# Second mixture of a fused attention and two-mixture kernel: three alternations a pair instead of eight

## The reference, cut to what matters

```python
def _moe2_ref(x, domain_probs, w1, w2):            # x 1536 x 384, w1 4 x 384 x 1024, w2 4 x 1024 x 384
    p = domain_probs / (domain_probs.sum(-1, keepdims=True) + 1e-09)
    out = np.zeros((N, D), dtype=np.float32)
    for e in range(E):
        h = np.maximum(x @ w1[e], 0.0)
        out += p[:, e:e + 1] * (h @ w2[e])
    return out.astype(np.float32)
```

## Time and profile before

| what | value |
|---|---|
| median of three runs | 683.82 us (683.36 to 684.65) |
| the profiled execution, its own time | 683.49 us |
| its span, first to last instruction | 681.8 us |
| outside the span | 1.7 us |
| PE busy | 673.4 us (99%) |
| DVE, POOL, ACT busy | 474.0, 327.6, 266.5 us |
| chain that ended last, by engine | PE 92%, SPq 4%, DVE 2% |
| granted TensorE clock | 1.00 of full speed |

### The profile page before, as it was taken

One profiled execution on the slowest core, in us unless ns is written; L12 is line 12 of the kernel. 1 busy time (PEld: TensorE's weight loads), 2 busy tenths in 40 slices (PEclk: granted clock), 3 DMA queues, 4 the chain that ended last, 5 costly groups with the idle time before them and its releaser, 6 DMA issues.

```text
span 681.8 us, 10695 instructions
## 1 busy us (share of the span) xinstructions
PE 673.4 (99%) x3915; PEld 625.5 (92%) x3915; DVE 474.0 (70%) x844; ACT 266.5 (39%) x485; POOL 327.6 (48%) x416
## 2 busy tenths in 40 slices
PE   8999999999999999999999999999999999999998
PEld 7789999999999999998999999999999999999997
DVE  6875748675676544019977967786778678867876
ACT  4525533223522352228534433343444344433430
POOL 4579561211111118870576458645854685467100
DMA  9997465006501001000020110011011101100003
GB/s 152 172 205 185 106 88 88 10 3 87 82 18 62 1 1 47 0 24 0 2 80 14 48 46 18 31 46 48 4 44 48 47 0 47 47 23 2 24 0 140
DMA packets 91911, 35.67 MB, mean 52 GB/s; under 512 B 73552, under 2 KB 91344, under 8 KB 91856
## 3 DMA queue, kind: packets, MB, share of 16 engines
q1 hardware_dynamic: 91408, 34.96, 23.2%
q10 hardware_dynamic: 448, 0.00, 0.0%
HBM read 32.00 MB, written 2.36 MB: 50 GB/s over the span
## 4 chain that ended last, share of the span: by engine, by line
PE 92%; SPq 4%; DVE 2%; DMA 1%; issue 1%; POOL 1%; ACT 0%; DVEq 0%
PE out_ps L1487 13%; PE out_ps L1489 13%; PE out_ps L1488 13%; PE hid_ps L1480 7%; PE hid_ps L1482 7%; PE hid_ps L1481 6%; PE at_ps L1743 5%; PE at_ps L1742 5%; PE at_ps L1741 4%; SPq L499 2%; PE hid_ps L1742 2%; PE hid_ps L1743 2%; PE hid_ps L1741 2%; PE at_ps L1580 1%; PE at_ps L1620 1%; PE out_ps L1742 1%
## 5 line engine op out<-in xcount | busy, mean ns | idle before, releaser
L1363 DVE SCALAR_TENSOR_TENSOR x<-out_ps,prob,x 128x384 f32<-128x384 f32 x180 | 110.2, 612 | 57.9 <-PE out_ps L1489 57.9
L1488 PE MATMUL out_ps<-early_r,late_r 128*128 128x384 f32 x384 | 129.4, 337 | 0.0
L1489 PE MATMUL out_ps<-early_r,late_r 128*128 128x384 f32 x384 | 129.3, 337 | 0.0
L1487 PE MATMUL out_ps<-early_r,late_r 128*128 128x384 f32 x384 | 129.0, 336 | 0.0
L747 POOL TENSOR_TENSOR hid_lo<-act_sb,hid_hi 128x384 fp32r<-128x384 f32 x44 | 44.9, 1019 | 152.5 <-ACT hid_hi L974 152.5
L1024 ACT COPY late<-at_ps 128x512 f32<-128x512 f32 x105 | 61.8, 589 | 101.8 <-PE at_ps L1743 98.7
L1487 PEld LDWEIGHTS out_ps<-early_r,late_r 128*128 128x128 f32 x384 | 72.1, 188 | 6.1 <-DVE x L1363 0.2
L1488 PEld LDWEIGHTS out_ps<-early_r,late_r 128*128 128x128 f32 x384 | 72.0, 188 | 5.6
L1329 DVE TENSOR_TENSOR act_sb<-hid_ps,act_sb 128x384 f32<-128x384 f32 x48 | 25.9, 541 | 71.1 <-PE hid_ps L1482 71.1
L1489 PEld LDWEIGHTS out_ps<-early_r,late_r 128*128 128x128 f32 x384 | 72.1, 188 | 0.0
L763 POOL TENSOR_TENSOR early<-stage 128x128 f32<-128x128 f32 x15 | 7.0, 465 | 102.1 <-PE at_ps L1743 102.1
(11 more groups left out here) (304 smaller groups left out, 1610.5 us busy)
## 6 DMA issues: line engine op xcount, KB each, us to landing
stage<-in_moe_w_dram SPq DMA_DIRECT2D x32, 384.0 KB, 3.4
stage<-in_moe_w_out_dram SPq DMA_DIRECT2D x4, 576.0 KB, 5.3
out_dram<-x SPq DMA_DIRECT2D x12, 192.0 KB, 1.9
stage<-in_moe_w_gate_dram SPq DMA_DIRECT2D x8, 216.0 KB, 4.2
stage<-in_moe_w_val_dram SPq DMA_DIRECT2D x8, 216.0 KB, 4.1
v_tm<-in_v_dram SPq DMA_DIRECT2D x9, 192.0 KB, 3.9
x<-in_alpha_dram SPq DMA_DIRECT2D x6, 288.0 KB, 4.9
a_tm<-in_alpha_dram SPq DMA_DIRECT2D x31, 48.0 KB, 2.3
```

Source lines behind the costliest of these rows:

```text
L1363: dve.scalar_tensor_tensor(out=a, in0=part, scalar=p, in1=a, op0=ALU.mult, op1=ALU.add).then_inc(s_acc, 1)
L1487: pe.matmul(dst, ah, bh, start=first, stop=False)
L1488: pe.matmul(dst, ah, bl, start=False, stop=False)
L1489: return pe.matmul(dst, al, bh, start=False, stop=last)
```

## The change: order of the tiles on PE, and what follows from it on DVE and ACT

On PE the output tiles of a pair stand in three runs instead of eight. The order is now A8 F6 E10, tiles 8 to 11 and 0, A7 C0 F13 B12, tiles 1 to 3, A14 D4 B1 A11, tiles 4 to 7, D2 C9 E3 B5. `LAG` is 8, and 6 for the last pair (`LAST_LAG`). Product 1 now stands ahead of product 11. On ACT, `keep(4)` stands behind the rounding of bank F. On DVE the sums are placed anew. No instruction is added or removed.

```diff
@@ -181,11 +181,11 @@
         V_EARLY = (0, 3, 10, 2, 4, 14, 5)
         V_LATE = {7: 1, 13: 3, 14: 4, 1: 5, 5: 7, 9: 8}
         V_DONE = (10, 0, 7, 13, 14, 4, 1, 2, 9, 3, 5)
-        MULS = (8, 6, 10, 7, 0, 13, 12, 14, 4, 11, 1, 2, 9, 3, 5)
+        MULS = (8, 6, 10, 7, 0, 13, 12, 14, 4, 1, 11, 2, 9, 3, 5)
         COPIES = (0, 8, 2, 6, 1, 4, 7, 9, 3, 5)
         ADDS = (7, 9, 0, 4, 2, 8, 3, 5, 1, 10, 6)
         BANKS = "FAECDB"
-        LAG = 9
+        LAG, LAST_LAG = 8, 6
 
         def nth(order, q, what):
             return len(order) * q + order.index(what) + 1
@@ -1050,12 +1050,12 @@
                     round_sum(5)
                 act.wait_ge(s_mul, nth(MULS, q, 12))
                 keep(1, bank_b)
-                act.wait_ge(s_mul, nth(MULS, q, 14))
-                keep(4, bank_a)
                 if pair > 1:
                     act.wait_ge(s_tile, NTILE * (pair - 1))
                 act.wait_ge(s_add, nth(ADDS, q, 9))
                 round_hidden(bank_f, pair, 1, 2)
+                act.wait_ge(s_mul, nth(MULS, q, 14))
+                keep(4, bank_a)
                 act.wait_ge(s_add, nth(ADDS, q, 0))
                 keep(7, bank_d)
                 act.wait_ge(s_add, nth(ADDS, q, 4))
@@ -1394,10 +1394,9 @@
             split_sum(14)
             split_plain(0, 5)
             split_sum(4)
-            add_up(0, 1)
             split_sum(1)
             split_sum(2)
-            add_up(0, 2)
+            add_up(0, 1)
             split_sum(9)
             split_sum(3)
             split_sum(5)
@@ -1411,28 +1410,32 @@
                 def split_bank(bank, f, t):
                     split_hidden(full_bank[bank], pair, BANKS.index(bank), f, t)
 
+                if q:
+                    add_up(pair - 1, 1)
                 dve.wait_ge(s_mul, nth(MULS, q, 13))
                 dve.wait_ge(s_copy, nth(COPIES, q, 1))
                 combine(bank_f, 1, ALU.subtract)
-                add_up(pair - 1, 3)
+                add_up(pair - 1, 2)
                 dve.wait_ge(s_add, nth(ADDS, q, 7))
                 dve.wait_ge(s_copy, nth(COPIES, q, 2))
                 combine(bank_f, 2, ALU.subtract)
-                add_up(pair - 1, 4)
+                add_up(pair - 1, 3)
+                split_bank("F", 1, 2)
                 dve.wait_ge(s_mul, nth(MULS, q, 4))
                 dve.wait_ge(s_copy, nth(COPIES, q, 4))
                 combine(bank_d, 4, ALU.subtract)
-                split_bank("F", 1, 2)
                 dve.wait_ge(s_mul, nth(MULS, q, 11))
                 dve.wait_ge(s_copy, nth(COPIES, q, 8))
                 combine(bank_a, 8, ALU.subtract)
-                add_up(pair - 1, 5)
+                add_up(pair - 1, 4)
                 dve.wait_ge(s_mul, nth(MULS, q, 10))
                 dve.wait_ge(s_copy, nth(COPIES, q, 7))
                 combine(bank_e, 7, ALU.subtract)
-                add_up(pair - 1, 6)
+                add_up(pair - 1, 5)
                 split_bank("A", 1, 0)
-                add_up(pair - 1, 7)
+                if pair < NPAIR - 1:
+                    add_up(pair - 1, 6)
+                    add_up(pair - 1, 7)
                 dve.wait_ge(s_mul, nth(MULS, q, 2))
                 combine(bank_d, 8, ALU.add)
                 dve.wait_ge(s_mul, nth(MULS, q, 9))
@@ -1441,34 +1444,30 @@
                 dve.wait_ge(s_copy, nth(COPIES, q, 3))
                 combine(bank_c, 3, ALU.subtract)
                 split_bank("E", 0, 0)
-                add_up(pair - 1, 8)
-                split_bank("C", 0, 2)
+                if pair == NPAIR - 1:
+                    add_up(pair - 1, 6)
                 dve.wait_ge(s_mul, nth(MULS, q, 5))
                 dve.wait_ge(s_copy, nth(COPIES, q, 5))
                 combine(bank_b, 6, ALU.subtract)
                 if pair == NPAIR - 1:
-                    add_up(pair - 1, 9)
+                    add_up(pair - 1, 7)
+                split_bank("C", 0, 2)
+                if pair == NPAIR - 1:
+                    add_up(pair - 1, 8)
                 dve.wait_ge(s_add, nth(ADDS, q, 8))
                 combine(bank_d, 5, ALU.add)
                 if pair < NPAIR - 1:
-                    add_up(pair - 1, 9)
-                add_up(pair - 1, 10)
+                    add_up(pair - 1, 8)
+                add_up(pair - 1, 9)
                 dve.wait_ge(s_add, nth(ADDS, q, 1))
                 dve.wait_ge(s_copy, nth(COPIES, q, 9))
                 combine(bank_b, 9, ALU.subtract)
-                if pair == NPAIR - 1:
-                    add_up(pair - 1, 11)
+                add_up(pair - 1, 10)
                 split_bank("D", 1, 1)
-                if pair < NPAIR - 1:
-                    add_up(pair - 1, 11)
-                else:
-                    add_up(pair, 0)
+                add_up(pair - 1, 11)
                 split_bank("B", 0, 1)
-                if pair < NPAIR - 1:
-                    add_up(pair, 0)
-                add_up(pair, 1)
-                add_up(pair, 2)
-            for t in range(3, NTILE):
+                add_up(pair, 0)
+            for t in range(1, NTILE):
                 add_up(NPAIR - 1, t)
 
         @block.tensor
@@ -1751,53 +1750,47 @@
                 pe.wait_ge(s_wu, q + 1)
                 bank_free("A")
                 mul(bank_a, 8, True)
-                if q:
-                    out_tile(last - 1, 9)
-                    out_tile(last - 1, 10)
                 bank_free("F")
                 mul(bank_f, 6, True)
-                if q:
-                    out_tile(last - 1, 11)
-                out_tile(last, 0)
                 bank_free("E")
                 mul(bank_e, 10, True)
+                if q:
+                    for t in range(LAG, NTILE):
+                        out_tile(last - 1, t)
+                out_tile(last, 0)
                 kept(0)
                 mul(bank_a, 7)
                 bank_free("C")
                 mul(bank_c, 0, True)
-                out_tile(last, 1)
-                out_tile(last, 2)
                 kept(8)
                 mul(bank_f, 13)
                 bank_free("B")
                 mul(bank_b, 12, True)
-                out_tile(last, 3)
+                for t in range(1, 4):
+                    out_tile(last, t)
                 kept(2)
                 mul(bank_a, 14)
-                out_tile(last, 4)
                 bank_free("D")
                 mul(bank_d, 4, True)
+                kept(1)
+                mul(bank_b, 1)
                 kept(4)
                 mul(bank_a, 11)
-                out_tile(last, 5)
-                out_tile(last, 6)
-                kept(1)
-                mul(bank_b, 1)
-                out_tile(last, 7)
+                for t in range(4, LAG if pair < NPAIR - 1 else LAST_LAG):
+                    out_tile(last, t)
                 kept(7)
                 mul(bank_d, 2)
                 kept(6)
                 mul(bank_c, 9)
                 kept(9)
                 mul(bank_e, 3)
-                out_tile(last, 8)
                 kept(3)
                 mul(bank_b, 5)
 
             hidden_plain(0)
             for pair in range(PLAIN, NPAIR):
                 sums_and_outputs(pair)
-            for t in range(LAG, NTILE):
+            for t in range(LAST_LAG, NTILE):
                 out_tile(NPAIR - 2, t)
             for t in range(NTILE):
                 out_tile(NPAIR - 1, t)
```

## The result

Over 21 runs of each, the changed kernel takes 684.71 us (684.06 to 685.6), the kernel before 683.55 us (683.08 to 684.65). The ratio is 1.0017, with an interval from 1.0011 to 1.0023. The change costs 1.16 us. One of the twelve executions of v2, a kernel further down, took 1337.61 us, a slow one; its ratio leaves it out.

The account below looks back on a forecast made before the run. PE, busy 99%, was taken as the bound, so only time between its matmuls counts. Steady pairs -0.6, pair 1's wait +1.35, the end +0.1: +0.85 us on 683.82, stated as 684.6 us; range 683.0 to 686.2.

Parts of the forecast that it names:

- the gain of the steady pairs: PE's steady pairs: loss falls from 0.353 to 0.31 us, gaining 0.04 a pair, 0.6 us over 15 pairs.
- The loss of 0.353 us a pair: PE, steady pair: 23.033 us against 22.68 of undisturbed steps, all lost at switches between tiles and products.
- Part 1: PE's three alternations for eight: long runs lose 0.067 us each, 0.20 a pair; gain 0.15, from 0 to 0.235.
- Part 2: PE's longer tile runs: six tiles wait closely for DVE's sums, costing 0.05 + 0.06 us a pair; bounds 0 and 0.36.
- Part 3: Product A11, pair 1: ACT's rounding of bank F delays the copy of state 4; PE waits 1.35 us, bounds 0 to 1.74.
- Part 4: Start costs 0 us; at the end six tiles instead of three meet DVE's backlog, 0.1 us more, from -0.3 to +0.5.
- A: Tile runs on PE: margin gone, close tiles stall, 2 to 4 us over 15 pairs, 686.6 to 688 us; chance 0.14.
- B: PE's steady pairs: switches give more, tile waits cost less; 681.8 to 682.0 us, with half of it 683.6; chance 0.12.
- C: PE: switches not the cause, or loss moves with the matmuls; only pair 1's wait stays, 685.2 us; chance 0.10.
- D: Pair 1, A11: ACT's rounding of bank F does not hold the copy, no wait, 683.3 us; chance 0.06.
- The rule of the Trainium skill: PE's matmul gap is N / 2.4 + 2.5 ns by its own columns alone, so switches cost nothing; this is C.
- The signs: POOL's period 22.95 to 23.02 us, seven products 4.80, A11 near 332.5 behind PE's only wait, F's rounding near 331.3.

Follow-up runs that it names:

- v2: The kernel before with tiles in six runs of two, products in runs of two, two, two, two, four, three, and DVE's sum of tile 7 moved: 682.14 us.
- e3: The changed kernel with ACT's copy of state 4 first again and DVE's sums cut to 256 of 384 columns, output incomplete: 680.85 us, ratio 0.9961.
- e4: The kernel before with DVE's sums cut to 256 of 384 columns, one third of the output left out: 682.54 us, ratio 0.9990.
- v4: The kernel before with product runs of two, five times, and one of five; tile 7's sum, bank E's combination and state 9's copy moved: 681.88 us.
- e1: The changed kernel with ACT's copy of state 4 again ahead of the rounding of bank F, in every pair: 684.03 us, ratio to before 1.0007.

## Why the prediction was right

The forecast was 684.6 us and +0.85; measured are 684.71 and +1.16. The mechanism held in each part, and one term, the gain of the steady pairs, was mis-sized. That 684.6 comes so near 684.71 is luck: it starts from 683.82, three runs' median, where 21 runs have 683.55, and so 0.27 too high makes up for a change 0.31 too low. The sum 683.82 + 0.85 is also 684.67 and not 684.6. Step by step:

- **The loss of 0.353 us a pair sits at the switches.** Shown. e3, e4, v2 and v4 have three, eight, six and six runs of products, and all four periods come out at 22.68 plus the sum of the prices.
- **Part 1, a long run costs no more than one of three.** Shown for runs of four, five and seven: 0.04 us in the run and 0.026 in the tile behind it.
- **Part 2, the tile waits give back 0.11 us.** Right in kind, too small. Taken from the mean lengths of the three tile runs over the pairs (5.315, 4.218 and 3.162 against 5.226, 4.186 and 3.146), it is 0.089 + 0.032 + 0.016 = 0.137. With 0.20 for the switches that makes a period of 23.017, measured 23.022. The saving is 0.01 us a pair and not 0.04, 0.15 us in all and not 0.6. Of this mis-sized term the larger part is the run of five: I had charged 0.11 for all six close tiles, and it alone takes 0.089.
- **Part 3, the wait of A11 in pair 1.** 1.33 us for 1.35, and the long step behind it, 0.11, which wasn't in the sum. What I hadn't seen is that it covers another: with ACT's order restored PE meets DVE's lateness at a tile and keeps half the loss (e1).
- **Part 4, the end.** The steps behind the last product lose 0.65 us instead of 0.62. I had charged 0.1.
- **The rivals.** A asked for a period above 23.04 and B for one below 22.87; it is 23.02. C has a total as near as the forecast's own (+1.45 and +0.85 for +1.16), for a wrong reason: e3 against e4 excludes it, since fewer switches do shorten the period. The range was said to leave out the upper half of A; from 686.2 up it leaves out all of it. D is excluded by the wait in the list.
- **The rule of the Trainium skill** (page "TensorE: Matmul & The Clock Gate", section "Back-to-back issue gap"). A gap that hangs on a matmul's own columns alone would make before, e3, v2 and v4 equal in period. They are 23.03, 22.88, 22.95 and 22.91. The page gives N / 2.4 + 2.5 ns for a single matmul taken by itself, which the prediction didn't say.
- **The signs.** The run of seven takes 4.80 us, A11's wait is PE's only one in the list, and A11 and ACT's rounding of F start at 332.5 and 331.4 once the 0.55 us ahead of pair 1 are taken off, for 332.5 and 331.3. The period was to be 22.95 to 23.02: its mean of 23.022 is at the very edge, and that of pairs 2 to 7, 23.033, outside. It is also under the 23.04 that would have spoken for A.

The sum closes by the stretches of PE: pair 1 costs 1.36 (1.46 in the run of A11, less 0.10 in its other runs), pairs 2 to 14 save 0.15, and pair 15 with what stands behind it saves 0.05, which makes 1.16.

## What to carry to other kernels

A PE that is busy for 99% can still lose 1.5% between its matmuls, and no list of waits shows it: measure the steps, multiply them out over a period, and compare. When work is put into longer runs to save switches, check the chain that must close within a run (matmul, sum, matmul through two banks) against the run's own pace; here runs of two tiles waited for nothing, and longer runs gave nearly all of the saving back. Before an in-order engine gets two instructions exchanged, look at the first round of the loop, where their releasers still lag.

## What the runs showed of the hardware

- The step of a matmul depends on what stood before. At 512 columns, the nine steps behind 384-column matmuls take 0.229, 0.233, 0.236, 0.224, 0.231, 0.236, 0.228, 0.232 and 0.231 us, and 0.2267 from then on. At 384 columns, the six behind 512-column ones add up to 1.066 us instead of 1.04 after nine steps or more, to 1.062 after three and to 1.044 after six. It is the same in all kernels here. Why six steps are kinder than three or nine I can't say.
- A semaphore that arrives in time can still cost. In the last run of tiles of the kernel before, and in the long runs after, a sum that ended 0.22 to 0.23 us ahead of the start of the matmul waiting for it made no gap, but often, not each time, 0.178, 0.185, 0.176 and 0.182 came again among the next steps, 0.03 us in all. Where the sum ended 0.24 us ahead or more, they mostly didn't. With the short sums of e3 these steps are gone.
